# 47-point transforms in four parts of TensorE's array, with the loads, stores and tiles around them moved

## The reference, cut to what matters

```python
X = np.fft.rfft(x, axis=1)                       # x: (2, 3008, 256) float32, 3008 = 47 * 64
Yr, Yi = Xr @ w_r - Xi @ w_i + b_r, Xr @ w_i + Xi @ w_r + b_i
Yr, Yi = soft_threshold(Yr, 0.01), soft_threshold(Yi, 0.01)
x = np.fft.irfft(Yr + 1j * Yi, n=3008, axis=1).reshape(6016, 256)
h = x @ w_in;  x = (max(h, 0) + alpha * min(h, 0)) @ w_out        # 256 -> 2048 -> 256
h = x @ w_in2; x = where(h >= 1, h, where(h <= -1, 0, (h + 1)**2 / 4)) @ w_out2
```

## Time and profile before

| | us |
|---|---|
| three runs, median (lowest to highest) | 1176.46 (1176.19 to 1177.62) |
| the profiled execution, its own time | 1175.93 |
| span of its trace, first to last instruction | 1173.8 |
| TensorE busy in the span | 1167.1 (99%) |
| VectorE, ScalarE, GpSimd busy | 887.2, 852.6, 687.0 |
| head: start to the first weight load of step 0 | 31.2 |
| first weight load of the mixing | 34.35 |

### The profile page before, as it was taken

One profiled execution on the slowest core, in us unless ns is written; L12 is line 12 of the kernel. 1 busy time (PEld: TensorE's weight loads), 2 busy tenths in 40 slices (PEclk: granted clock), 3 DMA queues, 4 the chain that ended last, 5 costly groups with the idle time before them and its releaser, 6 DMA issues.

```text
span 1173.8 us, 20998 instructions
## 1 busy us (share of the span) xinstructions
PE 1167.1 (99%) x6946; PEld 1138.4 (97%) x6946; DVE 887.2 (76%) x1678; ACT 852.6 (73%) x1880; POOL 687.0 (59%) x718
## 2 busy tenths in 40 slices
PE   9999999999999999999999999999999999999998
PEld 3899999999999999999999999999999999999998
DVE  4787777777777777777777787778778787878776
ACT  3445567777676777777677688888888787878776
POOL 1017647577565767666556566665757575756554
PEclk9999999999999999999999999999999999999999
DMA  9788411111121201202005500000000000000000
GB/s 354 228 258 267 153 55 44 52 42 54 54 70 40 68 28 41 95 27 68 19 5 177 197 19 2 27 1 28 1 28 1 27 1 27 1 27 1 14 15 27
DMA packets 41644, 77.61 MB, mean 66 GB/s; under 512 B 4672, under 2 KB 21184, under 8 KB 41536
## 3 DMA queue, kind: packets, MB, share of 16 engines
q1 hardware_dynamic: 38784, 67.82, 17.5%
q10 hardware_dynamic: 2752, 8.45, 2.0%
HBM read 45.97 MB, written 30.28 MB: 65 GB/s over the span
## 4 chain that ended last, share of the span: by engine, by line
PE 99%; DVE 0%; DMA 0%; issue 0%; SPq 0%; ACT 0%
PE bank L1272 45%; PE bank L1180 39%; PE bank L1146 6%; PE bank L1165 2%; PE bank L1120 2%; PE bank L1156 2%; PE bank L1131 2%; DMA x_sb<-x 0%; DVE g_sb L985 0%; DVE y_sum L881 0%; DVE bank L970 0%; DVE y_tile L1007 0%; ACT xc_hi L653 0%; DVE r L905 0%; DVE bank L975 0%
## 5 line engine op out<-in xcount | busy, mean ns | idle before, releaser
L519 POOL TENSOR_TENSOR g_lo<-g_sb,g_hi 128x376 fp32r<-128x376 f32 x510 | 505.4, 1002 | 362.5 <-ACT g_hi L784 361.6
L1272 PE MATMUL bank<-g_hi,w_out_hi 128*128 128x376 f32 x1024 | 342.8, 335 | 0.0
L1272 PE MATMUL bank<-g_hi,w_out_lo 128*128 128x376 f32 x1024 | 341.5, 333 | 0.0
L1180 PE MATMUL bank<-xc_hi,w_in_hi 128*128 128x376 f32 x896 | 302.5, 338 | 0.1
L1180 PE MATMUL bank<-xc_hi,w_in_lo 128*128 128x376 f32 x896 | 299.6, 334 | 0.0
L1180 PE MATMUL bank<-xc_lo,w_in_hi 128*128 128x376 f32 x896 | 299.0, 334 | 0.0
L784 ACT ACTIVATE g_hi<-g_sb 128x376 fp32r<-128x376 f32 x512 | 261.1, 510 | 45.6 <-DVE g_sb L985 28.7
L1272 PE MATMUL bank<-g_lo,w_out_hi 128*128 128x376 f32 x1024 | 259.6, 334 | 0.0
L1272 PEld LDWEIGHTS bank<-g_hi,w_out_hi 128*128 128x128 f32 x1024 | 192.2, 188 | 0.5
L1272 PEld LDWEIGHTS bank<-g_hi,w_out_lo 128*128 128x128 f32 x1024 | 192.7, 188 | 0.0
L1272 PEld LDWEIGHTS bank<-g_lo,w_out_hi 128*128 128x128 f32 x1024 | 184.2, 188 | 0.0
(11 more groups left out here) (84 smaller groups left out, 1528.8 us busy)
## 6 DMA issues: line engine op xcount, KB each, us to landing
gc<-group_consts SPq DMA_DIRECT2D x24, 256.0 KB, 4.5
zt<-slots_scratch SPq DMA_DIRECT2D x24, 256.0 KB, 4.0
inverse_scratch<-v_sb SPq DMA_DIRECT2D x24, 256.0 KB, 3.3
ut<-inverse_scratch SPq DMA_DIRECT2D x16, 384.0 KB, 5.1
slots_scratch<-a_sb ACTq DMA_DIRECT2D x15, 384.0 KB, 5.6
out<-y_tile SPq DMA_DIRECT2D x30, 188.0 KB, 1.9
x_sb<-x SPq DMA_DIRECT2D x17, 256.0 KB, 6.8
prep_raw<-wpack SPq DMA_DIRECT2D x16, 256.0 KB, 2.9
```

The lines of the kernel that those rows point to most:

```text
L519: pool.tensor_tensor(g_lo[kind][:, :], g_sb[n % 3][:, :], g_hi[kind][:, :].bitcast(f32), ALU.subtract)\
L1180: done = pe.matmul(bank_of[:, 0:N], w_part[:, fp, w * P:(w + 1) * P], x_part[q % 2][:, xs, :], start=first and n == 0, stop=last_one and n ...
L1272: last = pe.matmul(acc_bank[k][c][:, 0:N], w[:, fp, upper * D + c * P:upper * D + (c + 1) * P], g_part[kind][:, :], start=first and n == 0 ...
```

## The change

The padded 96 x 96 matrix of the 47-point transform, which held two interleaved copies of the 47-point matrix for two halves of the rows, becomes one matrix of 64 x 64 held twice, in partitions 0 to 63 and 64 to 127 (`fwd_sb`, 128 x 64). A tile of x now has one half of its rows in partitions 0 to 63 and the other in 64 to 127. `real47` makes four float32 matmuls of 64 x 512 instead of two of 96 x 512: for each half of the rows (h) one for each half of the columns (c). The built program gives each a quarter of the array, 64 rows by 64 columns, at (64h, 64c). Both of one h write one PSUM bank, so a bank holds half the rows and all columns of a tile in 128 partitions.

The stores are split by slot of the transform (`SLOTS_OF_PART`): part 0 (64 partitions) and part 1 (32 partitions), for two tiles at once, in two DRAM tensors. Step 0 only waits for part 0 of batch 0; part 1 of batch 0 is stored in steps 2 to 5, batch 1 in steps 6 to 17. The values are read for four steps at a time (`az_quads`, 512 KB in two DMAs, `QUAD_SLOTS` 2). Eleven tiles are transformed ahead of step 0 (batch 0 and three of batch 1), tile 11 at step 0 and tiles 12 to 15 at steps 2 to 5. The loads of tiles 8 and 9 wait until three of the four stores of batch 0's part 0 have landed, those of tiles 10 to 15 stand behind the first read of values. The mixing weights and the bias are loaded by SyncE ahead of that wait. The two half loads of tile 0 become one. The rows of the 64-point matrices are permuted to fit (on the host).

```diff
-FIRST_TILES = TILES - 1
-LATE_TILES = {1: FIRST_TILES}
-LATE_STORES = {2 * n + 2: TILES_PER_BATCH + n for n in range(TILES_PER_BATCH)}
+QUARTER = P // 2
+FIRST_TILES = TILES_PER_BATCH + 3
+LATE_TILES = {0: 11, 2: 12, 3: 13, 4: 14, 5: 15}
+LATE_STORES = {2 + n: (2 * n, 1) for n in range(4)}
+LATE_STORES.update({6 + 2 * n: (TILES_PER_BATCH + 2 * n, 0) for n in range(4)})
+LATE_STORES.update({14 + n: (TILES_PER_BATCH + 2 * n, 1) for n in range(4)})
+SLOTS_OF_PART = (QUARTER // 2, QUARTER // 4)
...
+        def store_a(eng, t, part):
+
+            b, q = divmod(t, TILES_PER_BATCH)
+            eng.wait_ge(a_left, t + 2)
+            eng.wait_ge(a_right, t + 2)
+            partitions = PARTS[part][2]
+            eng.dma_start(az_rows[part][b, :, q * HALF_COLS * 2:(q + 2) * HALF_COLS * 2], a_sb[partitions, t:t + 2, :])\
+               .then_inc(a_last_stored if (t, part) == (TILES_PER_BATCH - 2, 0) else a_stored[b][part], 16)
...
-            def load_values(p):
-                if p >= SLOTS:
-                    sp.wait_ge(b_done, 2 * p - 4)
-                sp.dma_start(zt[p % SLOTS][:, :, :], az_pairs[p, :, :, :]).then_inc(zt_in[p % SLOTS], 16)
+            def load_values(n):
+                if n >= QUAD_SLOTS:
+                    sp.wait_ge(b_done, 4 * (n - QUAD_SLOTS) + 4)
+                b, h = divmod(n, QUADS // 2)
+                part = int(h >= SLOTS_OF_PART[0] // 8)
+                if n and h in (0, SLOTS_OF_PART[0] // 8):
+                    sp.wait_ge(a_stored[b][part], 16 * TILES_PER_BATCH // 2)
+                for c in range(2):
+                    sp.dma_start(zt[n % QUAD_SLOTS][c * QUARTER:(c + 1) * QUARTER, :, :],
+                                 az_quads[part][b, c, h - part * SLOTS_OF_PART[0] // 8, :, :, :])\
+                      .then_inc(zt_in[n % QUAD_SLOTS], 16)
...
             load_matrices(0)
-            load_x(TILES - 2)
...
-            sp.wait_ge(a_stored[0], 16 * (TILES_PER_BATCH + 1))
+            sp.dma_start(wm_raw[:, :], wmix).then_inc(wm_in, 16)
+            sp.dma_start(bias_sb[:, :], bias).then_inc(bias_in, 16)
+            sp.wait_ge(a_stored[0][0], 16 * (TILES_PER_BATCH // 2 - 1))
+            load_x(TILES_PER_BATCH)
+            load_x(TILES_PER_BATCH + 1)
+            sp.wait_ge(a_last_stored, 16)
             load_values(0)
...
+            for t in range(TILES_PER_BATCH + 2, TILES):
+                load_x(t)
+                if t in (12, 14):
+                    load_matrices(t // 2 - 5)
+            load_values(1)
...
             def real47(t, banks):
-                for part, copied in enumerate((a_left, a_right)):
...
-                    pe.matmul(banks[part][0:ROWS_PAD, :], fwd_sb[:, :], x_tile(t)[:, part * HALF_COLS:(part + 1) * HALF_COLS],
-                              start=True, stop=True).then_inc(a_done, 1)
+                pe.wait_ge(x_in[t], 16 if t < FULL_TILES else 32)
+                for h, copied in enumerate((a_left, a_right)):
                     if t >= 2:
                         pe.wait_ge(copied, t - 1 if t < FIRST_TILES else t)
+                    rows = slice(QUARTER * h, QUARTER * (h + 1))
+                    for c in range(2):
+                        last = pe.matmul(banks[h][QUARTER * c:QUARTER * (c + 1), :], fwd_sb[rows, :],
+                                         x_tile(t)[rows, c * HALF_COLS:(c + 1) * HALF_COLS], start=True, stop=True)
+                    last.then_inc(a_done, 1)
```

More of the change, by code:

```diff
@@ L69 @@
 GC_SLOTS = 4
+QUADS, QUAD_SLOTS = STEPS // 4, 2
 P1_BY_SCALAR = 2
@@ L139, in fft_mix_ffn_kernel @@
     ACT = mybir.ActivationFunctionType
-    az = nc.dram_tensor("slots_scratch", [BATCH, SCRATCH_ROWS, D], f32, kind="Internal").ap()
+    az = [nc.dram_tensor(f"slots_scratch{part}", [BATCH, 2 * count * J, D], f32, kind="Internal").ap()
+          for part, count in enumerate(SLOTS_OF_PART)]
     win_z = nc.dram_tensor("w_in_scratch", [FP, 2, P, W * P], f32, kind="Internal").ap()
@@ L179, in fft_mix_ffn_kernel @@
         gc = [sb(f"gc{i}", [P, 4 * P], scope=fft) for i in range(GC_SLOTS)]
-        zt = [sb(f"zt{i}", [P, 2, D], scope=fft) for i in range(SLOTS)]
+        zt = [sb(f"zt{i}", [P, 4, D], scope=fft) for i in range(QUAD_SLOTS)]
         wm_hi = sb("wm_hi", [P, 4 * D], f32r, fft)
@@ L230, in fft_mix_ffn_kernel @@
         a_right = sem("a_right")
-        a_stored = [sem(f"a_stored{i}") for i in range(BATCH)]
-        zt_in = [sem(f"zt_in{i}") for i in range(SLOTS)]
+        a_stored = [[sem(f"a_stored{i}{part}") for part in range(2)] for i in range(BATCH)]
+        zt_in = [sem(f"zt_in{i}") for i in range(QUAD_SLOTS)]
+        a_last_stored = sem("a_last_stored")
         gc_in = [sem(f"gc_in{i}") for i in range(GC_SLOTS)]
@@ L608, in _ @@
                 copy_a(t, a_bank[(2 * t) % 4])
-                if t < TILES_PER_BATCH:
-                    store_a(t)
-                if t >= LEAD and t + LEAD in SCALAR_LOADS:
-                    load_rows(act, t + LEAD, 1)
-                if t == TILES_PER_BATCH:
-                    act.dma_start(wm_raw[:, :], wmix).then_inc(wm_in, 16)
+                if t < TILES_PER_BATCH and t % 2 == 0 and t:
+                    store_a(act, t - 2, 0)
+                if t == TILES_PER_BATCH - 1:
+                    store_a(act, t - 1, 0)
+                    for late in range(TILES_PER_BATCH, SCALAR_LOADS):
+                        load_rows(act, late, 1)
             act.wait_ge(wm_in, 16)
@@ L640, in weights_hi @@
                     if n == 0:
-                        act.wait_ge(a_stored[1], 16 * TILES_PER_BATCH)
+                        for part in range(2):
+                            act.wait_ge(a_stored[1][part], 16 * TILES_PER_BATCH // 2)
                     act.wait_ge(s_made, n + 1)
@@ L1279, in _ @@
             for t in range(FIRST_TILES):
-                real47(t, [a_bank[(2 * t + part) % 4] for part in range(2)])
+                real47(t, [a_bank[(2 * t + h) % 4] for h in range(HALVES)])
             for s in range(STEPS):
```

85 lines of the change are left out of this document (31 added, 54 removed).

## The result

The changed kernel takes 1180.98 us, median of 8 runs (1180.33 to 1181.92), against 1176.20 us of 8 runs of the kernel before on the same chip (1175.73 to 1177.62): 1.0040 times as long, 95% interval 1.0029 to 1.0051. The forecast was 1175.0 with a range of 1171.5 to 1180.5. The profiled execution took 1181.37 us with a span of 1179.2, 5.4 more than before's 1173.8.

What follows compares the result with a forecast made beforehand. TensorE was taken as the bound, with DMA also near its limit in the head. Mixing earlier -5.2, late tiles +3.1, array changes +0.8 gave -1.3 us; forecast 1175.0, range 1171.5 to 1180.5.

Steps and rivals of the forecast that it cites:

- So I cost all this at nothing; it is hidden behind the steps' matmuls: DMAs behind step 0 (tiles, matrices, second values, part 1 of batch 0): all hidden behind matmuls, 0 us.
- If the cover failed, a late quad would stall by the latency it lacks, 3 to 4 us once: DMAs behind step 0: the stall if values for four steps came late, 3 to 4 us, not in the sum.
- Reading four steps at a time moves the same bytes on the same release: nothing: Reads of values in the steps: going to four steps at a time costs 0 us.
- 227 GB/s of the 415 that they could: DMA rate in the steps, taken as leaving room enough to cost the DMAs behind step 0 at nothing.
- Mixing begins at 29.15: End of the head: the first mixing starts at 29.15 instead of 34.35, 5.2 us earlier.
- the gain would be 0.4 us larger: Tiles 8 to 10 in the head: without the halved clock, tile 10 would only wait for data, gaining 0.4 us.
- Late tiles: Tiles 12 to 15 in steps 2 to 5: 3.1 us given back, plus 0.8 for eight array changes at 0.1.
- Two quarters at a time: Rival on TensorE: only neighbours overlap, a tile takes 1.71 us; +3.9 to +5.6, 1180.4 to 1182 us; chance 0.15.
- The bytes alone bound: Rival on the head: bytes move without holes, mixing starts 6.8 us earlier; about -3, 1173.3 us; chance 0.34.
- No overlap: Rival on TensorE: quarters never run together, 3.42 us a tile; +26, 1202 us; chance 0.04.

Runs made afterwards that it cites:

- e5: Changed kernel with values and matrices of the next two steps ahead of weight loads and token reads in SyncE's list: 1178.94 us against before's 1177.26 (1.0012).
- e2: Changed kernel with values read two steps at a time into three slots of 256 KB: 1180.06 us against before's 1176.92 (1.0022).
- e1: Changed kernel with three slots for four-step reads of values instead of two, each read four steps sooner: 1183.38 us against before's 1176.92 (1.0053).
- e15: Kernel before the change, with only values and matrices put ahead of weights and tokens in SyncE's list: 1176.32 us against 1177.36 (0.9997).
- e3: Changed kernel with two whole-array 128x512 matmuls per tile instead of four in quarters, transform left out: 1188.08 us against before's 1176.92 (1.0100).
- e9: Changed kernel in e5's order, fifteen tiles ahead, x waiting only for its buffer, mixing weights behind the last store: 1178.32 us against before's 1176.31 (1.0009).
- e13: e12 with fourteen tiles ahead and the x of the last two asked for behind the first values: 1175.02 us against before's 1176.51 (0.9987).
- e12: e9 with values read two steps at a time instead of four: 1176.59 us against before's 1176.51 (0.9996).
- e14: Changed kernel in e5's order with eight tiles ahead, all x of batch 1 behind the first values: 1180.84 us against before's 1176.51 (1.0036).
- e10: e9 with fourteen tiles ahead, tile 14 at step 0 and tile 15 at step 1: 1178.83 us (1.0016 of before).
- e6: e5 with first matrices, mixing weights and bias issued by ScalarE behind the last store of batch 0's part 0: 1180.75 us against before's 1177.26 (1.0030).
- e7: e6 with seven idle products on TensorE behind tile 7 to hold the clock: 1180.65 us (1.0028 of before).

## Why the prediction was wrong

The sign was wrong: forecast -1.3 us against the profiled execution before, measured +5.4. Three terms make up the 6.7 between, 2.3 + 0.5 + 3.9. The largest alone would not have turned the sign: without it the sum is still +1.5, as e5 has it (1.0012).

**"So I cost all this at nothing; it is hidden behind the steps' matmuls"**: the step that failed, 3.9 us. The mechanism stood in the text ("If the cover failed, a late quad would stall by the latency it lacks, 3 to 4 us once"), with 0.03 for all unseen stalls. "Reading four steps at a time moves the same bytes on the same release: nothing" was wrong. Bytes, requests and their size are the same (24 of 256 KB, before and after), but two of them now stand in a row and put 512 KB and 1.25 us of issuing ahead of the matrices, in a list where the last entry had 0.1 us to spare. From step 6 to step 47 e5 takes all of it away (100.72 us against before's 100.74 and the changed kernel's 104.69), e2 takes 1.0, e1 0.3; e15 shows that the kernel before had just enough slack. The reasoning behind it was a rate, "227 GB/s of the 415 that they could". The earlier trace rows itself had the share of the DMA engines at 0.72 for those 227, which is 315 at a full share, not 415, and the earlier trace rows, which the text reads as 402 to 418 from 7 us on, has 365 at 0.94 and 354 at 1.00 among them. And it was read in other steps than those that matter: in those before step 20 the kernel before was at 0.94 with 286. An average was no cover for a request that has to be in time.

**"Mixing begins at 29.15"**: it began at 31.43, 2.3 late. Of this 1.8 is tile 10, and that is its x: asked for at 21.87 and there at 27.17, where the forecast had 25.0 by pricing everything in flight at 415 GB/s; the stretch of 23 to 25 us moved 255 at a share of 1.10. Tile 8, put down at the 3.1 to 3.3 us of a DMA with room, came 1.3 late in 4.3. The other 0.5 is the copy: the four quarters' records end nearly together, so ScalarE's copy of tile 10 began 1.1 us after the tile and not 0.6. From that copy to the mixing it took 3.09 us, forecast 3.15. Requests (19.0 and 20.4), idle TensorE, fallen clock and the pace of tiles 8 and 9 were right. Tile 7 ended at 14.9 and not at 13.3, and the last store was issued at 15.7 and not at 14.2; it landed at 20.5 all the same, where the text had 20.3 from the bytes in flight. The 0.7 us of latency in that 20.3 stands in no row and was not measured by itself. Of the clock the text said that without the fall "the gain would be 0.4 us larger"; the landing of tile 10's x at 27.17, behind the end of tile 9 at 27.0, shows that it would have been nothing.

**Late tiles**: forecast 3.1 + 0.8 = 3.9, measured 4.43. The price of a quarter tile was right (0.86), and so was the doubt about the borders; their size was taken at 0.1 each, where the two cost 0.34 together, the whole of the 0.165 of tail each time. The Trainium skill, page "TensorEngine Tiling (Array Packing)", Key Properties, says that a change of mode drains the array. The trace fits it, with 1.20 a late tile against 0.86 in a row and e3's 1.71 without a border.

**The rivals.** "Two quarters at a time" gave 1180.4 to 1182, and the time fell in that range by luck: eight records take 0.86 us and not 1.71, so this one is out. The Trainium skill's sentence that matmuls "themselves stay in program order" (page "TensorE: Matmul & The Clock Gate", Part 2) was taken there to keep the quarters apart; the trace shows that it doesn't, and agrees with the concurrent matmuls of Part 3 of that page. A time that agrees with a rival does not speak for it. "The bytes alone bound" was right in that the head is bound by transfers: e9 has its tiles done five microseconds before its values. But the bytes are not all of one price, so it gave 1173.3 where the closest, e13, has 1175.0. "No overlap" (3.42 us a tile) is out by the same 0.86.

**What stays open.** Why the engines move 216 to 292 GB/s at shares of about 1 when values are under way. The values are read in rows of 1 KB and x in rows of 4 KB, and the low rate is seen in the stretches of e9, e12, e13 and e14 as well. The Trainium skill, page "DMA: Bandwidth & Descriptors", Specifications, gives 512 B as the least transfer for line rate. By that both kinds of rows should reach it, and 255 GB/s at a share of 1.10 doesn't look so. But no run read the values in rows of another length, so that the row's length is the cause is argued, not shown; it may be the mixture, or that they were written just before. Low rates at high shares are seen without values too: 277 at 0.90 in the changed kernel from 19 to 21 us, with values asked for only at 20.51, and 221 at 0.91 in the earlier trace rows from 3 to 5 us. Open also is what the clock costs in e9 and e10, since neither was run with it held.

## What to carry to other kernels

Before a read is made larger, find what is issued behind it on the same queue and by how much that lands ahead of its use: the slack of the last entry in the list (here 0.1 us) decides, not the average share of the DMA engines. When a wait is put down to one of several loads, look up when each of them landed. Read share and rate of a stretch together; the rate at a share of 1 is what the kinds of transfer in that stretch can reach, and a rate from a stretch of large rows doesn't price one of small ones. Halving an engine's work in a stretch where the transfers are also near their limit buys only what the transfers leave, and moving work out of such a stretch into one that the engine bounds is paid in full, borders included (here 4.43 us for four tiles).

## What was not expected of the hardware

Four float32 products in the quarters of the array, of two records each, ran side by side though the two records of a product share a quarter: a tile each 0.86 us instead of 1.71. The two changes between quarters and the whole array around a late tile cost 0.34 us together. From the first request for values to step 0 it took 4.9 us with the DMA engines nearly idle before (e14), and 6.2, 8.6 and 9.7 beside streams of x (e13, e12, e9). The granted clock of the changed kernel was 0.54 from 25 to 27 us and 1.00 from 27, with tiles 8 and 9 (16 records) between 23.3 and 27.0; TensorE's second waits in e6, e7 and e9 (4.3, 4.2 and 5.2 us) were followed by a tile at 1.99 us instead of 1.09.
